# A fused attention and two-layer expert kernel: the values products of an older pair of heads moved into the middle of the even slot's first-layer products, ahead of the new pair's scores

## The reference, cut to what matters

```python
# attention: batch 4, 8 heads, 768 tokens, head width 64; a window of 128 keys and 4 sink keys
scores = q @ k.T / sqrt(64); scores[not kept] = -1e9
a = exp(scores - max); a = a / (sum(a) + 1e-9)
x = (a @ v) heads side by side            # 3072 tokens x 512
# first two-layer block
h = x @ w_in                              # 512 x 2048
x = (h - tanh(h)) @ w_out                 # 2048 x 512
# expert block: each token goes to one of 8 experts
e = argmax(x @ w_gate + bias[modality]); p = its softmax probability
out = p * (relu(x @ w1[e]) @ w2[e])       # 512 x 1024, 1024 x 512
```

## Time and profile before

| what | value |
|---|---|
| median of 3 runs | 1076.66 us (1076.42 to 1077.22) |
| the profiled execution's own time | 1072.89 us |
| its span, first to last instruction | 1071.3 us |
| PE busy | 993.2 us, 93% of the span |
| DVE, ACT, POOL busy | 649.5, 581.6, 327.6 us |
| windows 0 to 6 with their attention work | from about 91 to 705 us |

### The profile page before, as it was taken

How to read it: one execution, slowest core, us unless ns; L and a number is a source line. 1 busy time by engine, 2 the same in 40 slices (tenths; PEclk the granted TensorE clock), 3 DMA queues, 4 the chain that set the end, 5 groups by cost and what they waited for, 6 DMA issues and landing times.

```text
span 1071.3 us, 23847 instructions
## 1 busy us (share of the span) xinstructions
PE 993.2 (93%) x7968; PEld 607.1 (57%) x7968; DVE 649.5 (61%) x2272; ACT 581.6 (54%) x1329; POOL 327.6 (31%) x462
## 2 busy tenths in 40 slices
PE   1757998999999999999999999999899999899996
PEld 0524444555554565555455555555487777677773
DVE  5665767667767767777866775646765334633331
ACT  3767777666657765766666675536422224522221
POOL 4776675112116211213511210101122322232322
PEclk9858999999999999999999999999999999999998
DMA  8710001201100220100110010041025111111111
GB/s 308 262 35 19 18 19 65 78 19 36 48 18 19 63 80 19 49 18 19 37 48 19 22 45 1 2 166 51 1 51 183 68 54 47 40 40 49 49 49 38
DMA packets 24375, 60.30 MB, mean 56 GB/s; under 512 B 9504, under 2 KB 9760, under 8 KB 22752
## 3 DMA queue, kind: packets, MB, share of 16 engines
q1 hardware_dynamic: 15392, 45.77, 12.7%
q0 software_dynamic: 5728, 13.43, 4.0%
q10 hardware_dynamic: 3168, 0.02, 0.2%
HBM read 45.35 MB, written 14.12 MB: 56 GB/s over the span
## 4 chain that ended last, share of the span: by engine, by line
PE 74%; DVE 11%; ACT 6%; issue 5%; POOL 2%; DVEq 1%; DMA 0%; ACTq 0%; SPq 0%; POOLq 0%
PE h_ps L751 18%; PE acc L807 18%; PE s_ps L1856 6%; PE h_ps L1907 6%; PE pt_ps L1856 6%; PE acc L1907 5%; PE pt_ps L639 3%; PE s_ps L569 3%; PE x_out L706 2%; ACT probs L587 1%; PE s_ps L858 1%; DVE pt_lo L648 1%; DVE qk_top L401 1%; PE pt_ps L662 1%; PE x_out L1833 1%
## 5 line engine op out<-in xcount | busy, mean ns | idle before, releaser
L807 PE MATMUL acc<-w_out_all,g_hi 128*128 128x512 f16 x768 | 228.4, 379 | 0.0
L751 PE MATMUL h_ps<-xt_hi,w_in_all 128*128 128x384 f16 x960 | 196.4, 327 | 4.6 <-DVE g_raw L772 3.0
L807 PE MATMUL acc<-w_out_all,g_lo 128*128 128x512 f16 x384 | 146.0, 380 | 3.3 <-DVE g_lo L792 2.7
L751 PEld LDWEIGHTS h_ps<-xt_hi,w_in_all 128*128 128x128 f16 x960 | 91.2, 100 | 62.3 <-issue 7.0
L807 PEld LDWEIGHTS acc<-w_out_all,g_hi 128*128 128x128 f16 x768 | 75.1, 98 | 77.7
L763 ACT ACTIVATE g_raw<-h_ps,batch_scale 128x384 f32<-128x384 f32 x120 | 69.7, 581 | 88.5 <-PE h_ps L751 84.5
L792 DVE SCALAR_TENSOR_TENSOR g_lo<-g_raw,batch_scale,g_hi 128x384 f16<-128x384 f32 x128 | 84.7, 662 | 44.5 <-ACT g_hi L782 44.5
L782 ACT ACTIVATE g_hi<-g_raw,batch_scale 128x384 f16<-128x384 f32 x128 | 77.9, 608 | 55.3 <-DVE g_raw L772 53.8
L101 POOL TENSOR_TENSOR tick<-tick 1x1 f32<-1x1 f32 x83 | 15.5, 187 | 295.4 <-ACT y L1923 117.5
L751 PE MATMUL h_ps<-xt_lo,w_in_all 128*128 128x384 f16 x480 | 98.3, 328 | 0.0
L580 DVE CUSTOM_DVE_ANT_0 probs<-s_ps,mask 128x260 f32<-128x260 f32 (+1 forms) x192 | 70.2, 402 | 45.5 <-issue 38.1
(11 more groups left out here) (315 smaller groups left out, 2104.9 us busy)
## 6 DMA issues: line engine op xcount, KB each, us to landing
qk_raw<-in_qk SPq DMA_DIRECT2D x31, 454.0 KB, 3.4
raw<-in_w SPq DMA_DIRECT2D x16, 512.0 KB, 8.5
v_raw<-in_v SPq DMA_DIRECT2D x4, 1536.0 KB, 7.9
x_tokens<-x SPq DMA_DIRECT2D x24, 256.0 KB, 2.5
w_in_all<-in_w_in SPq DMA_DIRECT2D x4, 1024.0 KB, 9.6
w_out_all<-in_w_out SPq DMA_DIRECT2D x4, 1024.0 KB, 9.9
x_tokens<-g_raw SPq DMA_DIRECT2D x1, 1024.0 KB, 12.4
vs_raw<-in_v SPq DMA_DIRECT2D x24, 4.0 KB
```

Source lines behind the costliest of these rows:

```text
L751: mm = eng.matmul(h_of(m, f), w16[0][:, f, x * DM + k * P:x * DM + (k + 1) * P], r[:, par, k, :], start=(i == 0), stop=(i == 3 * KD - 1))
L807: mm = eng.matmul(acc[t][:, :], l[f % 2][:, t * P:(t + 1) * P], w16[1][:, f, x * DM:(x + 1) * DM], start=(f == 0 and i == 0), stop=(f == N ...
```

## The change

`weigh_values` of the older pair no longer follows the 12 first-layer products of an even slot. It stands in `between`, after the first eight of them and directly ahead of the new pair's scores. In the very last even slot, where there are no first-layer products, `between` is now called by itself; only the values products could be there, and no pair is left for them.

```diff
@@ window(E, eng, w), PE's part
                     def between():
                         if even:
+                            stage(weigh_values, E, eng, ago(4))
                             stage(score_pair, E, eng, ago(0))
                             stage(transpose_probs, E, eng, ago(2))
...
                         if nxt:
                             mlp_in(E, eng, *nxt, between)
-                        stage(weigh_values, E, eng, ago(4))
+                        else:
+                            between()
```

## The result

| | before | changed |
|---|---|---|
| median of 4 runs | 1076.54 us (1074.49 to 1077.22) | 1089.76 us (1087.34 to 1090.40) |
| the profiled execution's own time | 1072.89 us | 1089.44 us |
| its span | 1071.3 us | 1087.8 us |

The change makes the kernel slower: the ratio is 1.0132, with a 95% interval of 1.0117 to 1.0147, or 13.2 us on the medians. The forecast was 1085.0 us, 8.45 us of loss.

What follows compares the result with a forecast made beforehand. PE's list plus any wait put into it bounds the kernel. Terms 4.1 + 1.2 + 0.75 + 1.5 + 2.0 - 1.1 + 0.6 - 0.6 = 8.45 us on 1076.66 gave 1085.0 us; 8-in-10 range 1077.5 to 1091.

Steps and rivals of the forecast that it cites:

- The shift: Slots 0, 8, 16 and 24 (t = 2 values products): `h_ps` and ACT's list behind it 0.78 us later.
- Scores behind the routing copy: Slot 10, windows 1 to 6: scores wait for ACT's `x2t`, 0.78 or 0.58 us each, 4.1 us lost.
- The turn behind `normed`: Slots 2, 18, 26: PE's turn waits for `normed`, 0.13 us in nine slots of windows 1 to 6, 1.2 us lost.
- Slot 18 of windows 2 and 4: Turn's copy, tanh and gate 0.4 us late; PE loses 0.37 us twice, 0.75 us in all.
- The sinks' low half in slot 24: Moved values products wait for DVE's line 671: 0.25 us three times, 0.38 us twice, 1.5 us lost.
- Shapes and the covered logit: One change of shape fewer in twelve slots, 1.1 us gained; scores' wait for the logit covered twice, 0.6 us gained.
- The sinks' slots: Slots 6, 14, 22 and 30: turn follows products of another shape, 0.6 us lost over 16 slots.
- Window 0: Four slots with t = 2 values products: bounds 0 and 3.1 us, 2.0 us of loss taken.
- (a): Only the shapes count, PE never waits for the chain behind the tanh: 1075.0 to 1076.1 us, chance 0.12.
- (b): Only the routing copy's 4.1 us counts; turns, sinks and window 0 have room: 1079 to 1081 us, chance 0.09.
- (d): Absorbed: PE's delays shorten its present waits, half the loss or more taken back: 1077 to 1080 us, chance 0.09.
- (c): Snowball: delays build up, PE waits in most of 28 t = 2 slots, 0.5 us each: 1090 to 1100 us, chance 0.10.

Runs made afterwards that it cites:

- e3: The change, but only t = 2 values products moved, between the new scores and the last four first-layer products: 1083.22 us, ratio 1.0083 to the kernel before.
- e4: t = 2 slots without a turn: all twelve first-layer products, then scores, then values products; other pairs as before: 1070.71 us, ratio 0.9971 to the kernel before.
- e1: The change, but only t = 0 and t = 1 values products ahead of the scores: 1075.30 us, ratio 1.0011 to the kernel before.
- e8: The change in windows 1 to 6 only, window 0 in its old order: 1082.55 us, ratio 1.0072 to the kernel before.
- e6: The change, but only t = 0 values products ahead of the scores: 1073.98 us, ratio 0.9995 to the kernel before.
- e7: e4's order in t = 2 slots, plus t = 0 values products ahead of the scores except in slot 20: 1070.13 us, ratio 0.9956 to the kernel before.
- e9: e7, but window 0's t = 0 values products left at the end of their slots: 1067.85 us, ratio 0.9946 to the kernel before.
- e5: The change, but ACT does an odd slot's conversion only after the next even slot's exps: 1098.87 us, ratio 1.0225 to the kernel before.
- e2: The change, but only t = 2 values products ahead of the scores: 1087.79 us, ratio 1.0131 to the kernel before.

## Why the prediction held, point by point

**The bound** was read rightly: PE's list plus the waits put into it. PE's busy time hardly moved, and its waits did.

**The shift** had the right place and cause (e3 against e4) and was too small. I took 0.78 us, because the last four first-layer products "lose their own 0.10 us step". That step lies behind them: tanh follows their start by 0.86 us with or without it, so the shift is the full 0.88 us. Of every room that is used up, 0.10 us more was lost.

**Scores behind the routing copy**: 4.1 us forecast, 4.7 measured; 0.78 and 0.58 became 0.88 and 0.69. The group of waits came to 5.0 us, as forecast.

**The turn behind `normed`**: 1.2 us forecast, 2.35 measured: 2.15 in the nine slots counted, and 0.2 in slot 4 of window 1, which the count had missed. 0.13 became 0.22 (0.31 in slot 26 of windows 2 and 4): room 0.71, less the lag 0.06, against a shift of 0.88 instead of 0.78. Window 4, slot 2, of the changed kernel, ACT and PE, against the earlier trace rows:

```profile
463.73 0.92 ACT L607 ACTIVATE normed<-probs,row_sum 128x260 f32<-128x260 f32 x2 [0.38 <-DVE row_sum L600]
...
464.69 0.66 PE L639 MATMUL pt_ps<-ident,normed 128*128 128x128 f32 x4
```

**Slot 18 of windows 2 and 4**: 0.37 us each forecast, 0.90 measured (0.68 there and 0.22 in slot 20). I had the turn's copy, tanh and gate 0.4 us late. DVE's low half is indeed 0.40 us late (3.56 us from the slot's start for 3.16), but the gate is 0.75 us late, since DVE operations stand between the two. DVE before:

```profile
325.77 0.69 DVE L648 TENSOR_TENSOR pt_lo<-pt_ps,pt_hi 128x512 f16<-128x512 f32 x1 [0.30 <-ACT pt_hi L644]
326.37 0.17 DVE L887 TENSOR_TENSOR logit<-logit,iota_e 128x24 f32<-128x24 f32 x1
```

and of the changed kernel, DVE and POOL:

```profile
334.42 0.69 DVE L648 TENSOR_TENSOR pt_lo<-pt_ps,pt_hi 128x512 f16<-128x512 f32 x1 [0.60 <-ACT pt_hi L644]
334.58 0.92 POOL L450 TENSOR_TENSOR q_lo<-qk_raw,q_hi 128x384 f16<-128x384 f32 x1
335.03 0.51 DVE L887 TENSOR_TENSOR logit<-logit,iota_e 128x24 f32<-128x24 f32 x1
...
335.79 0.62 DVE L772 SCALAR_TENSOR_TENSOR g_raw<-h_ps,batch_scale,g_raw 128x384 f32<-128x384 f32 x1
```

The shifted chains of DVE and POOL meet: an addition of 0.17 us takes 0.51, to just behind the end of POOL's subtraction (335.50). The prediction had looked at POOL and found "nothing new that I find close".

**The sinks' low half in slot 24**: 1.5 us forecast (0.25 and 0.38), 1.4 measured (0.23 and 0.35). Window 3, DVE and PE, against the earlier trace rows:

```profile
437.20 0.54 DVE L671 TENSOR_TENSOR pt_hi<-pt_ps,pt_hi 32x384 f16<-32x384 f32 x1
437.80 0.35 PE L706 MATMUL x_out<-pt_lo,v_hi 128*64 128x256 f16 x4 [0.16 <-DVE pt_hi L671]
```

**Shapes and the covered logit**: 1.7 us of gain forecast, 1.5 measured. PE in slot 12 of window 2, against the earlier trace rows, has no step left between first- and second-layer products (0.65 us), and the scores no longer wait:

```profile
314.25 0.28 PE L569 MATMUL s_ps<-k_hi,q_lo 64*128 64x260 f16 x2
...
315.17 0.81 PE L751 MATMUL h_ps<-xt_hi,w_in_all 128*128 128x384 f16 x4
315.82 0.38 PE L807 MATMUL acc<-w_out_all,g_lo 128*128 128x512 f16 x1
```

**The sinks' slots**: 0.6 us lost forecast, 0.9 measured. That "the nine sinks waits do not move" was only roughly so: they grew by 0.9 us in windows 1 to 6, and e1 shows why.

**Window 0** is the term that was sized worst: 2.0 us taken, 4.2 by the slots and 6.4 by e8, above the 3.1 us that I had called the upper bound. That bound counted t = 2 slots times the shift. It left out that one late list is met at more than one place (the turn, the gate and the sinks in different slots), the later turn behind t = 0 values products (e6), and POOL, which the prediction gave "slots of room" and for whose weights PE waits 0.9 us longer in slot 28.

All in all windows 1 to 6 cost 9.5 us where the terms gave 6.45, and window 0 did the rest: 13.2 us for 8.45. That puts the time near the top of the range: the path and the direction were right, but nearly every loss was taken too small, and it is the width of the range, 6 us above the forecast, that takes in the sum's error of 4.8 us. **The rivals**: (a) is out, since the chain had no room (by its own terms its upper bound was 1075.6 us, not 1076.1); (b) is out, since turns, sinks and window 0 cost together more than the routing copy; (d) is out, since PE's waits did not shrink. (c) had the direction of the error, but not its form: the delays do not build on each other, they are one shift of 0.88 us that reaches PE where the room is smaller.

**Left open**: window 0 was not taken apart slot by slot with kernels of its own, and the 2 us between its slots and its share of the medians are within what the two intervals leave uncertain. That line 887 was stretched by POOL is read from the traces of this case (below) and was not tried by a kernel that moves POOL alone.

## What to carry to other kernels

When a piece of work is moved ahead on the busiest engine, price what is pushed back, not what is moved: here 0.79 us of products cost nothing in most of their own slots and up to 0.88 us a slot or two later, because the product that completes `h_ps` opens the longest in-order list of another engine. So put the products that feed such a list first, fill up behind them with the work whose readers have room, and keep products of one array shape together (e4, e7, e9). Where a list is already back to back, taking one operation out of it to relieve one wait can cost more at the next place (e5), so compare two kernels slot by slot and not by the wait that one has in mind.

## What the runs showed of the hardware

**A DVE operation stretched by POOL.** DVE's addition at line 887 reads two tensors in SBUF, 128x24. In windows 2 and 4 of before, e1, e4, e6, e7 and e9 it took 0.17 to 0.19 us; there POOL was at a TENSOR_SCALAR (line 492) or just changing to it. In e5 it took 0.17 us with POOL idle. In windows 2 and 4 of the change, e2, e3 and e8 it fell into POOL's TENSOR_TENSOR (line 450) each time and took 0.50 to 0.51 us, ending 0.04 us behind it: eight of eight. Neighbours on DVE under the same POOL work, the low half (line 648, 0.69 us in both kernels) and the gate (line 772, 0.62 us), read PSUM and kept their time where they ran beside POOL's TENSOR_TENSOR; `g_lo` (line 792), also with two inputs in SBUF, takes 0.62 us alone and up to 1.23 us beside it in the kernel before already, 1.60 us in the changed one. The Trainium skill, SBUF — State Buffer, Who interferes with whom, states that DVE and GpSimd share a pair of ports under an exclusive lock, and that a DVE operation with two SBUF inputs contends with GpSimd's reads, while one with at most one, outside the two-port modes, does not. The traces agree, with 0.17 against 0.51 us; no kernel was run that moves POOL's operation alone.

**A change of array shape on PE** costs about 0.1 us between f16 products of this kernel, and adds up: 25 slots with one fewer gave 0.10 to 0.14 us each (e4).

**The early rise of the clock differs between executions.** After 92 us the granted clock was 1.00 in some profiled executions (before, e2, e4, e5, e6, e8) and 0.51 to 0.77 in others (the change, e1, e3, e7, e9) for the next 6 us, with up to 2.7 us in the first slot of window 0 (e1). Single executions also fell to 0.50 for a few us later on: e1 in slot 24 of window 4, e5 in slot 16 of windows 2 and 4, with 1.5 to 1.6 us in each such slot. A difference of 2 us between two single profiles says nothing here.
